# Expert slots of two sizes and a later normalisation in a recurrence + SoLU + top-2 mixture kernel

## The reference

```python
# 1. complex-decay linear recurrence, for every batch and head
a_n = a * min(|a|, 0.999) / (|a| + 1e-6)            # complex a = a_re + i a_im
for t in range(S):
    S_re, S_im = Re(a_n[t] * S) + outer(k[t], v[t]), Im(a_n[t] * S)
    y[t] = q[t] @ S_re
x = y as (3072, 384)
# 2. one dense layer, d_ff = 1024
h = x @ w_in
z = h * softmax(h)
x = (z - mean(z)) / sqrt(var(z) + 1e-6) * g_ln @ w_out
# 3. mixture of E=8 experts, F=1024, two experts a token
noisy = x @ w_gate + log1p(exp(x @ w_noise)) * noise
for the top-2 experts e of each token, with softmax weights w:
    out += w * (relu(x @ w1[e]) @ w2[e])
```

## Time and profile before

| | |
|---|---|
| three runs | 1179.08, 1179.63, 1182.27 us; median 1179.63 |
| the profiled execution | 1182.65 us, its span 1180.9 us |
| first phase | 0 to 622.8 us of the span |
| 31 slots | 622.8 to 1169.4 us |
| after the last matmul | about 11.5 us |
| PE / DVE / ACT / POOL busy | 89% / 73% / 55% / 39% of the span |

### The profile page before, as it was taken

One profiled execution on the slowest core, in us unless ns is written; L12 is line 12 of the kernel. 1 busy time (PEld: TensorE's weight loads), 2 busy tenths in 40 slices (PEclk: granted clock), 3 DMA queues, 4 the chain that ended last, 5 costly groups with the idle time before them and its releaser, 6 DMA issues.

```text
span 1180.9 us, 21982 instructions
## 1 busy us (share of the span) xinstructions
PE 1046.8 (89%) x7898; PEld 983.2 (83%) x7898; DVE 857.6 (73%) x1592; ACT 647.9 (55%) x1105; POOL 459.4 (39%) x413
## 2 busy tenths in 40 slices
PE   0467789989999999999939999999999999999996
PEld 0256678877887888888739999999999999999995
DVE  5799788988888899646445777676676676676672
ACT  6733856756756745645524555555555555555551
POOL 4011233344444443434531443453453453454342
PEclk9868888989999999999968999999999999999998
DMA  9430121231221211222216667676676676776740
GB/s 260 152 101 21 41 88 31 65 88 28 68 89 28 68 36 54 49 55 64 98 28 246 230 210 266 237 234 237 229 254 247 238 246 214 237 256 206 231 142 1
DMA packets 85980, 167.51 MB, mean 142 GB/s; under 512 B 18566, under 2 KB 57696, under 8 KB 85872
## 3 DMA queue, kind: packets, MB, share of 16 engines
q1 hardware_dynamic: 72336, 137.61, 36.3%
q0 software_dynamic: 13440, 28.40, 6.5%
q10 hardware_dynamic: 96, 0.10, 0.0%
HBM read 148.83 MB, written 21.92 MB: 145 GB/s over the span
## 4 chain that ended last, share of the span: by engine, by line
PE 59%; DVE 2%; ACT 1%; issue 1%; DMA 1%; POOL 0%; POOLq 0%; DVEq 0%; ACTq 0%; SPq 0%
PE bank L1412 23%; PE bank L1609 22%; PE bank L1473 4%; PE bank L1521 4%; PE bank L1403 3%; PE bank L1495 1%; PE bank L1533 1%; ACT z L943 1%; ACT x2t L938 0%; PE bank L1510 0%; DVE w1l L1145 0%; DMA xg<-xs,mine 0%; DMA tags<-tag,idx 0%; DVE zl L1247 0%; PE bank L1553 0%
## 5 line engine op out<-in xcount | busy, mean ns | idle before, releaser
L975 ACT ACTIVATE hh<-bank 128x256 fp32r<-128x256 f32 x248 | 95.4, 385 | 256.3 <-PE bank L1412 256.3
L1412 PE MATMUL bank<-sxh,w1h 128*128 128x256 f32 x744 | 212.0, 285 | 2.1 <-DVE sxl L1362 2.1
L1412 PE MATMUL bank<-sxh,w1l 128*128 128x256 f32 x744 | 210.3, 283 | 0.0
L1412 PE MATMUL bank<-sxl,w1h 128*128 128x256 f32 x744 | 210.0, 282 | 0.0
L1381 DVE SCALAR_TENSOR_TENSOR hl<-bank,hh 128x256 fp32r<-128x256 f32 x248 | 105.0, 423 | 120.5 <-ACT hh L975 120.5
L697 POOL DMA_INDIRECT out<-yo,mine x62 | 77.5, 1250 | 279.0 <-DVE yo L1374 261.1
L1609 PE MATMUL bank<-w2h,hh 128*128 128x384 f32 x496 | 167.4, 337 | 0.0
L1609 PE MATMUL bank<-w2l,hh 128*128 128x384 f32 x496 | 166.8, 336 | 0.0
L1609 PE MATMUL bank<-w2h,hl 128*128 128x384 f32 x496 | 166.6, 336 | 0.0
L1412 PEld LDWEIGHTS bank<-sxh,w1h 128*128 128x128 f32 x744 | 140.8, 189 | 2.5 <-DVE sxl L1362 2.5
L1412 PEld LDWEIGHTS bank<-sxh,w1l 128*128 128x128 f32 x744 | 141.5, 190 | 0.0
(11 more groups left out here) (202 smaller groups left out, 2328.4 us busy)
## 6 DMA issues: line engine op xcount, KB each, us to landing
raw<-in_w SPq DMA_DIRECT2D x62, 1536.0 KB, 7.6
ar<-in_a_re SPq DMA_DIRECT2D x6, 768.0 KB, 4.7
turn<-in_a_im SPq DMA_DIRECT2D x6, 768.0 KB, 5.9
qk<-in_q SPq DMA_DIRECT2D x48, 96.0 KB, 2.4
qk<-in_k SPq DMA_DIRECT2D x48, 96.0 KB, 2.5
out<-wide SPq DMA_DIRECT2D x9, 512.0 KB, 11.5
vt<-in_v SPq DMA_DIRECT2D x24, 192.0 KB, 2.7
xs<-x SPq DMA_DIRECT2D x24, 192.0 KB, 2.8
```

What stands on the lines that cost most here:

```text
L975: nc.scalar.activation(hh[:, f % NH, :], bank[:, f % 2, 0:CAP], ACT.Relu).then_inc(hh_done, 1)
L1412: ins = MM(dst, stationary[a_](cc), moving[b_](cc), start=(n_ == 0), stop=(n_ == len(terms) - 1))
```

## The change

Tiles: in rounds b = 2 `norm` goes behind the maximum and `fill(1)`; in rounds b = 3 it goes behind the SoLU product and the state addition. The table `FILLS` spreads the product pieces otherwise: in chunks after the first, b = 0 has two more ahead of the reciprocal and two fewer ahead of `xl`, b = 2 has 8, 1, 2, 1, 3, 4 pieces for 9, 1, 4, 1, 2, 2; for the first chunk b = 3 has four ahead of the maximum and nine behind, where all 13 were ahead. For the first chunk ACT's `squares(5)` goes behind the evacuation of y, and `inverse_squares` goes behind `x2_evac`.

Slots: there are still 31, but six of them (3, 8, 13, 18, 23, 28) are half slots of 128 rows. A half slot makes its hidden product the other way round (tokens stationary, 512 columns of w1 moving, two parts of 9 matmuls), writes the relu to `row_h`, transposes it back (8 transposes), and makes the result in 24 matmuls. `raw1` and `raw2` get two buffers each. POOL's order becomes partial(s), gather(s+3), give(s). Ahead of a half slot, ACT and DVE split w1 of the slot behind it at the end of the whole slot before it. The table of slots takes 24 small operations for 14.

```diff
-SLOTS = (2 * NTOK - (E - 1)) // CAP + E
+WHOLE, HALVES = 25, 6
+SLOTS = WHOLE + HALVES
+HALF_SLOTS = (3, 8, 13, 18, 23, 28)
...
+def give_block(s):
+    return max([GIVE] + [4 - (s - t) for t in HALF_SLOTS if t <= s])
...
-        FILLS = (((0, 0, 0, 0, 0, 0, 0), (0, 0, 0, 0, 0, 0, 16), (4, 1, 6, 1, 2, 12, 8), (13, 0, 0, 0, 0, 0, 0)),
-                 ((6, 1, 7, 1, 2, 5, 0), (12, 1, 3, 1, 2, 1, 0), (9, 1, 4, 1, 2, 2, 0), (2, 0, 0, 0, 0, 0, 0)))
+        FILLS = (((0, 0, 0, 0, 0, 0, 0), (0, 0, 0, 0, 0, 0, 16), (4, 1, 6, 1, 2, 12, 8), (4, 9, 0, 0, 0, 0, 0)),
+                 ((6, 1, 9, 1, 2, 3, 0), (12, 1, 3, 1, 2, 1, 0), (8, 1, 2, 1, 3, 4, 0), (2, 0, 0, 0, 0, 0, 0)))
...
             def load_w1(s):
...
-                apart(sp, (w1_lo, KC * s))
+                apart(sp, (w1_lo, KC * (s - 1)))
...
             for s in range(SLOTS):
-                if s + 2 < SLOTS:
-                    gather(s + 2, s % 2, (s + 2) % NM)
                 partial(s, s % 2, s % NM)
+                if s == 0:
+                    gather(2, 0, 2)
+                if s + 3 < SLOTS:
+                    gather(s + 3, (s + 3) % 2, (s + 3) % NM)
                 give(s, s % 2, s % NM)
...
+            def half_slot(s, par, more):          # ACT
...
+                row(0)
+                if more:
+                    tokens(s + 1, 1 - par)
+                row(1)
+                high(0)
+                high(1)
+                if more:
+                    for j_ in range(W2P):
+                        w2_piece(s + 1, 1 - par, j_)
...
-                if b == 2 and 0 < c < C - 2:      # DVE, ahead of the maximum
-                    norm(2 * c + 4)
...
-                if b == 3 and c + 2 < C:
-                    norm(2 * c + 5)
+                if b == 2 and 0 < c < C - 2:
+                    norm(2 * c + 4)
                 fill(2)
...
+                if b == 3 and c + 2 < C:          # behind the state addition
+                    norm(2 * c + 5)
...
+            def half_slot(s, par, more):          # DVE
...
+                if more:
+                    tokens(s + 1, 1 - par)
+                give(s - 1, 1 - par, (s - 1) % NM)
+                low(0)
+                low(1)
+                if more:
+                    for j_ in range(W2P):
+                        w2_piece(s + 1, 1 - par, j_)
...
+            def half_slot(s, par, more):          # PE
+
+                if more:
+                    tokens(s + 1, 1 - par)
+                half_hidden(s, par, 1)
+                half_turn(s, par, 0)
+                half_turn(s, par, 1)
+                if more:
+                    first_hidden(s + 1, 1 - par)
+                half_result(s, par, 0)
+                half_result(s, par, 1)
```

## The result

The changed kernel takes 1143.97 us, the median of four runs (1142.83 to 1146.41), against 1179.78 us for the kernel before on the same chip. The ratio is 0.9687, with a 95% interval from 0.9664 to 0.9709: 36 us faster, where 55.6 were forecast. The time lies 20 us above the point. It is inside the stated range, whose upper end is 1147, and outside the forecast's own bounds of 1110 to 1137.

What follows compares the result with a forecast made beforehand. It took the slots as bound by PE and the tiles by the order on DVE. From 1182.65 it took 15.5 (tiles) and 41.6 (slots), added 1.5 (start): 1127.1, less 3.0 for the median: 1124 us, range 1107 to 1147.

Steps and rivals of the forecast that it cites:

- rival 2: Half slots: they stumble on DVE's split work, 3 us more for each, 1142 us; chance 0.10.
- Rival 1: Tiles: they give nothing, as PE may be the bound and waits only change place, 1139.5 us; chance 0.11.
- PE work of a half slot: Slots: 9.62 us of PE work against 17.56 for a whole slot, 7.94 less each, 47.6 for six.
- rival 5: Slots: matmuls of 512 columns run at 0.175 us, the pace of those of 384, 5.7 less, 1118 us; chance 0.02.
- allowance of 0.7 us per half slot for the chain on POOL: Slots behind each half slot: late landings between gives hold DVE and partly PE; 0.7 us taken, bounds 0 and 3.
- Rival 4: Slots: POOL's give-to-give chain with exposed landings sets the pace, slower than before, 1202 us at landings of 14; chance 0.02.
- The tiles: Tile chunks: moving `norm` and pieces removes DVE's waits for `scale`, 15.5 us gained, bounds 5 and 22.
- The reciprocal's wait: Tiles, rounds b = 3: 2.6 of the 3.36 us idle ahead of `norm` stay as a wait for the exponential's sum.
- DVE's thin cover in the half slot: Half slots: DVE delivers both `low` and the next `hl` in time, with only 0.3 and 0.7 us to spare.
- The start: Start of the slots: the longer slot table delays slot 1's tags and weights, 1.5 us added, bounds 0 and 4.
- Rival 3: Slots: weights can't come faster, so the slots keep their time, 1166 us; chance 0.03.
- The tail: Behind the last slot: taken as unchanged.

Runs made afterwards that it cites:

- kernel without weights: Changed kernel without the raw w1 and w2 loads from slot 5 on, so those slots use stale weights: 1132.8 us (one run).
- kernel with eight tag buffers: Changed kernel with eight buffers for tags in place of six (NM = 8), no other edit: 1175.8 us, ratio 0.9954 to the kernel before.
- tile edits alone: Kernel before with all edits of the tiles and its old slots: 1178.8 us, ratio 0.9985 to the kernel before.
- long sums out of the way: POOL's two magnitude sums cut to 8 columns from the second chunk on: changed kernel 1125.6 us; with old tiles and new slots 1139.3 us.
- short sums: Changed kernel with POOL's two magnitude sums cut to 8 columns from the second chunk on: 1125.6 us, ratio 0.9538 to the kernel before.
- right behind `prev`: Changed kernel with each pair of weight loads held until POOL has issued `prev`: 1134.2 us, ratio 0.9598 to the kernel before.

## Why the prediction was right, and where its sum was off

**Direction and range.** The direction was right at both places, and so was the PE work. The point was 20 us low because two terms were mis-sized, and 1144.0 is outside the forecast's own 1110 to 1137. That it lies in the range is luck: the range reached to 1147 to take in rivals 1 and 2, and neither came true as written.

**PE work of a half slot: right.** Forecast 7.94 less 0.3 for each of six, 45.8 us. (Eight steps of 2.12 are 16.96, not 16.9, which changes nothing here; and the lower bound of 24 for the slots does not follow from its terms, which give 6 x (7.94 - 0.3 - 3) = 27.8.) The kernel without weights shows 523.4 - 479.3 = 44.1, or 7.35 each. The 512-column matmuls take 0.23 us as the earlier trace rows had it, which settles rival 5. The Trainium skill (TensorE: Matmul & The Clock Gate, Back-to-back issue gap) states 131 ns for such a matmul; the trace does not agree, with 0.23 us here as before.

**The allowance of 0.7 us per half slot for the chain on POOL: mis-sized.** It came to 4.2 us and measured 14.0. The step that failed is the landing of `prev`, taken as the 5.0 of the kernel before, with 0.4 us to spare in slots of 15.4. That was a landing in a kernel whose weight loads left at other moments. The double buffers move them, and I costed that edit by what it lets ACT do, not by what the transfers then collide with: `prev` now lands in 6.8. (No run has the half slots with single buffers, so that the double buffers alone do this is not shown.) DVE waited 19.9 us for it, PE 10.1 behind DVE, and the lower clock after the longest wait adds some 3.4.

The other landing in that chain was misread. The 5.2 of the earlier trace rows is a median over all transfers that touch `out`, the gathers `prev` and the fills at the start among them, and its 15.1 is one of these fills (512 KB, at 25.3 us), not a scatter. The trace of before has no landing of a scatter; that of the changed kernel has:

```profile
prev<-out,mine POOLq DMA_INDIRECT x56, 6.8
out<-yo,mine POOLq DMA_INDIRECT x56, 3.2
```

So the two landings are 10.0 us in sum where 10.2 was reckoned: the chain of 15.0 was right in the middle by luck, and what costs are the slots above it. The upper bound, 3 us per half slot, did hold. Rival 4 named this chain, but its price was for landings of 13.3 us in sum in every slot; in the changed kernel they reached that once (13.6). The kernel with eight tag buffers shows how near rival 4 was: 520.9 us of slots, almost the old time.

**The tiles: mis-sized.** 15.5 us forecast, 6.7 in the profiled execution, 3.6 in the mean of traces. The step that failed is "the idle 2.06 us goes; the rest of the round is DVE work of the same length", and its like for b = 3. The waits did go, all of them. The work did not keep its length: put into the time in which DVE used to stand still, it lay beside POOL's sums and was held. Two things show it: the hold grows by 12.7 us with the tile edits alone (40.9 to 53.6), and with the long sums out of the way old and new tiles differ by 7 to 14 us. The reciprocal's wait, put at 2.6 us for b = 3, is 0.75 or nothing: DVE comes later to it, in the one case held by the sum at 293.90. Rival 1 (PE is the bound) gave nearly the right time for the tiles. Its reason is not what limits them, since shorter sums make the chunks 4 to 5 us shorter. But the argument against it was weaker than I wrote: the chunk of 78 us ran at a granted clock of 1.00 and the one of 89 us at 0.92, and for as many matmuls (686) PE was busy 75.7 and 82.2 us. More than half of the 11 us between them went with the clock, which the prediction left out.

**DVE's thin cover in the half slot, rival 2: held.** Both `low` came in time, and PE's waits for `hl` come to 10.1 us in six places, with 5.1 us the longest: the size of the waits for `prev`, not of a half slot's hole.

**The start: +1.5 us forecast, +0.1 measured.** SP issued w1 of slot 1 at 612.85 us, 46.5 behind the last `xl`, against 44.2 before: 2.3 us later, as reckoned, and nobody waited for it. **Rival 3** (weights can't come faster) fell: ACT never waited for a raw weight, in slots down to 14.8 us. The tail, put at nothing, gave 1.6 us: from the issue of the last scatter to the end of the span there are 6.4 us (1136.18 to 1142.6), before 8.0.

**Open.** The same tile code ends between 566.4 and 572.3 us. The low clock goes with it, as said above, but which of the two drives the other is open, and so is the share of the clock in the gain of short sums. And only one exact place of the weight loads (right behind `prev`) was tried, which leaves 0.9 us to the slots without weights.

## What to carry to other kernels

A wait that you remove is replaced by work that now runs at that time: look what the other engines do in that window, and compare the durations of an instruction beside them and apart from them before you take its length as fixed. Before a transfer is made earlier by a second buffer, list the short transfers that other engines wait for, and decide which is issued first; a wait that looks like a nuisance can be what keeps the big load behind the small one. When a trace has a value twice (0.36 and 1.87 us for one line), the minimum and the maximum tell more than the mean. A landing time that is given for a tile can mix transfers of several kinds: ask for the one instruction whose landing the chain waits for. And compare the granted clock before you compare two stretches of PE.

## What the runs showed of the hardware

- A DVE operation with both inputs in SBUF that started while POOL's sum of two SBUF operands ran was held until that ended: 12 elements 1.84 us instead of 0.17, 192 elements 1.87 instead of 0.36. One that started 0.14 us ahead of the sum kept its 0.36 us. Operations with an input in PSUM (1.22, 1.28 us) were the same beside POOL.
- A scatter of 128 rows beside a weight load of 1.5 MB: POOL's wait for a scatter that was out over 4 us ahead of the next load was 2.45 us, and 5.97 and 6.18 with a load issued 0.5 us behind it. Being issued first by half a microsecond did not protect it.
- One change of a buffer count (six to eight for 2 KB of tags) cost 32 us, by releasing loads of 3 MB in another part of the slot.
- PE stood still for 5.1 us; from 1072.5 us on the granted clock was 0.50 for 6.8 us, and 21 matmuls fell into these 6.8 us (1.3 of them still idle), against 48 into the 6.7 us behind them at 1.00.
